# Two edits at the head of the routed blocks and one at the end of an attention, feed-forward and expert kernel

## The chip, the cores and the metric

The kernel runs on one core of a Trainium2 chip. The metric is the device time of one launch in microseconds (us). Engines are called by the names of the profile: PE is the matrix engine (PEld its weight loads), DVE is VectorE, ACT is ScalarE, POOL is GpSimd, and SP is SyncE, which here only issues transfers. A "q" behind the name of an engine (POOLq, DVEq, SPq) marks what its sequencer does alone: branches, register operations, waits, issues of transfers.

## The reference

Three stages follow one another on 2304 tokens (4 batches of 576) of 512 numbers, all in float32.

1. Attention of 8 heads of 64 with a causal window of 64 positions.
2. A dense feed-forward layer, 512 to 2048 to 512, with the activation h * tanh(softplus(h)).
3. A routed layer of 8 experts:

```python
do_compute = x @ w_skip > 0
xc = x[do_compute]
e_idx = argmax(xc @ w_gate)            # one expert of eight for each token
gate_w = softmax(xc @ w_gate)[e_idx]
for e in range(8):
    y[e_idx == e] = gate_w * (relu(xc @ w1[e]) @ w2[e])   # 512 -> 1024 -> 512
out = x;  out[do_compute] = xc + y
```

How many tokens an expert gets is known only on the chip, once the last token has been routed.

## The kernel before, in words

**Attention and dense layer** run in nine chunks of 256 tokens, each in eight ticks (`NC`, `NJ`); `tick(J)` of each engine says in which order it does its part. A chunk's result goes to `ytile`, SP stores it to `out` (`store_y`, line 407) and, with the gate in column 513, to the scratch tensor `y_rows` (`store_rows`, line 416). For each chunk the router finds expert and position of every token, and POOL scatters the token numbers into eight lists in DRAM (`scatter_tokens`, line 1505; `all_placed`, line 1516, waits until they have landed).

**Routed blocks.** A block is 128 tokens of one expert. PE makes the product with `w1` (`expert_up`, line 674, 64 matmuls of 128x128, 4 per 128 of the 1024 hidden numbers) in two halves, transposes the rows of the next block (`rows_T`, line 667, 4 matmuls), and makes the product with `w2` (`expert_down`, line 688). There `w2` and the hidden numbers are split into a rounded part and a rest (hi and lo), so that 24 matmuls of 128x512 add up in the bank `OB`. Around PE, in each engine's own order:

- ACT (`expert_block`, line 994) rounds the four quarters of `w2` (`split_w2`, line 872), makes the two halves of the ReLU (`expert_relu`, 886) and copies the next block's transposed rows (`rows_T_out`, 866).
- DVE (line 1427) takes the four rests of `w2` (`rest_of_w2`, 1240), the two rests of the ReLU (`rest_of_relu`, 1248), and writes gate times product plus row to `ot` (`gate_rows`, 1258).
- SP (`load_block`, line 433) reads the expert's number from a table in SBUF and issues two transfers of 2 MB: `w1` once the up product two blocks back is done (`bh_ok`), `w2` once the down product two blocks back is done (`bz_ok`). Each has two buffers, by the parity of the block. `w2_lo` lies over `w2`: the rests are written in place.
- POOL (line 1613) waits until the previous block's result has landed in `out` (`o_out`), loads the token numbers of the block three ahead (`load_tokens`, 1605), gathers the rows of the block two ahead into `xs` (`gather`, 1533), and scatters this block's result (`scatter_rows`, 1592). It does these one after the other.

**Blocks 0, 1 and 2 are early.** Their experts are picked before the last chunk is routed (`pick_first`, `pick_second`, `pick_third`, lines 1190 to 1238), on the experts' counts so far. So their weights and rows come while the last chunk is in work. All blocks from 3 on need the table `eid_i` and `row0_i`, which DVE computes after the last chunk (lines 1387 to 1422); the 20th step of the semaphore `tstep` says that it is there. Which expert each block has follows from the table; the experts that were not picked come in ascending order behind the early three.

**Order around the change.** SP (lines 470 to 488): `w1` of block 2; the last chunk's stores; `w2` of block 2 (after block 0's down product, since it goes to block 0's buffer); the wait for `tstep`; a wait for block 3's gathered rows (line 481); blocks 3 to 7; and then a loop over blocks 8 to 27, in which each block stands under a guard `If(i * RING + n < nblk)`, four guards to an iteration (`RING`), side by side. `nblk`, the number of blocks, is 12 on this input, so the loops of SP, PE, ACT, DVE and POOL run four iterations with sixteen false guards behind block 11. POOL (lines 1584 to 1624): the gather of block 2, the last chunk's token scatters, block 0's result, the wait that these tokens are placed, the wait for `tstep`, block 3's token numbers (1620), then `expert_block(1)`, with the numbers of block 4, the gather of block 3 and the result of block 1; behind the loop POOL waits for the landing of the last result (1624) and leaves. DVE, in the last tick (1300 to 1304), picks the third expert, takes two rests of block 1's `w2` and a rest of block 0's ReLU; then it copies the second half of the last chunk out of the bank `Y1` (1374, 1375), which PE's transposes and SP's stores wait for.

## Time and profile before

| what | us |
|---|---|
| median of three runs (722.07 to 725.32) | 723.67 |
| the profiled execution, its own time | 722.84 |
| span of the profiled execution, first to last instruction | 721.3 |
| of it, PE busy with matmuls (95%) | 684.9 |
| first matmul of the up product of block 2 | 565.32 |
| the same of block 4 | 604.14 |
| last matmul of block 11 begins | 709.22 |

All starts are counted from the start of the span. The time of an execution is 1.54 us more than its span. The mean granted clock of PE is 0.981 of full speed; a granted clock of 1.00 is 2.4 GHz and 0.50 is 1.2 GHz. A view called timeline lists instructions in order of their start, merged where they repeat; behind a row stands in brackets how long the engine had been idle and which instruction ended that. "Issue" there is time in which it waited for nothing that the profile shows.

### The profile page before, as it was taken

The numbers are of one execution on the slowest core, as the hardware profiler recorded it, in microseconds if no ns is written. First come the engines' busy times: TensorE is split into PE (matmuls) and PEld (weight loads), VectorE is DVE, ScalarE is ACT, GpSimd is POOL, SyncE is SP. The second block draws the span as 40 slices with busy tenths as digits, with TensorE's granted clock in tenths as the row PEclk, the third lists the DMA queues.
The fourth block names the chain that finished last, engine by engine and source line by source line (L and its number), as shares of the span: only waits on it lengthen the run. The fifth ranks groups of instructions, "written<-read, shape, count | busy, mean of one in ns | idle before, by whom it ended". The sixth has DMA issues, their size and how long they took to land. (4 is left out here: it accounts for less than half of the span.)

```text
span 721.3 us, 13783 instructions
## 1 busy us (share of the span) xinstructions
PE 684.9 (95%) x4958; PEld 605.2 (84%) x4958; DVE 489.0 (68%) x935; ACT 357.2 (50%) x784; POOL 253.7 (35%) x231
## 2 busy tenths in 40 slices
PE   5899999999999999999999999999999969999993
PEld 4776898888889888889889898988888868899992
DVE  5898767866866876785886785787788524364450
ACT  4546565555554654555555456544452323443430
POOL 4312434343443352443353353454652310221220
PEclk8999999999999999999999999999999998999998
DMA  9733221171164141232133124013477599999930
GB/s 273 236 117 118 74 67 37 39 126 44 37 119 98 48 96 37 75 70 63 42 91 75 37 46 124 1 31 94 174 289 217 163 393 333 343 330 354 349 126 2
DMA packets 62834, 97.16 MB, mean 135 GB/s; under 512 B 23014, under 2 KB 27110, under 8 KB 62768
## 3 DMA queue, kind: packets, MB, share of 16 engines
q1 hardware_dynamic: 59152, 91.01, 41.8%
q0 software_dynamic: 3168, 4.51, 1.9%
q10 hardware_dynamic: 448, 0.79, 0.4%
q8 instruction: 39, 0.64, 0.4%
q14 instruction: 27, 0.22, 0.2%
HBM read 84.97 MB, written 13.73 MB: 137 GB/s over the span
## 5 line engine op out<-in xcount | busy, mean ns | idle before, releaser
L1496 POOL TENSOR_TENSOR q_sb<-n_sb,r_sb 128x512 f32<-128x512 f32 x72 | 94.3, 1309 | 286.9 <-DVE a_sb L1101 162.9
L591 PE MATMUL Y<-wout_hi,g_hi 128*128 128x512 f32 x272 | 111.6, 410 | 3.2 <-ACT g_hi L845 3.0
L572 PE MATMUL H<-x_hi,win_hi 128*128 128x256 f32 x384 | 112.0, 292 | 2.0 <-DVE x_lo L1035 1.9
L572 PE MATMUL H<-x_hi,win_lo 128*128 128x256 f32 x384 | 108.4, 282 | 0.0
L572 PE MATMUL H<-x_lo,win_hi 128*128 128x256 f32 x384 | 108.4, 282 | 0.0
L591 PE MATMUL Y<-wout_lo,g_hi 128*128 128x512 f32 x272 | 107.3, 394 | 0.0
L684 PEld LDWEIGHTS H<-xT,w 128*128 128x128 f32 x768 | 89.2, 195 | 5.1 <-DMA w<-moe_w 4.2
L684 PE MATMUL H<-xT,w 128*128 128x128 f32 x768 | 89.7, 278 | 3.8 <-DMA w<-moe_w 3.8
L1502 POOL TENSOR_TENSOR g_lo<-g_sb,g_hi 128x512 fp32r<-128x512 f32 x68 | 88.3, 1298 | 2.5 <-ACT g_hi L845 1.9
L1081 DVE TENSOR_SCALAR u_sb<-e_sb 128x512 f32<-128x512 f32 x72 | 34.3, 476 | 71.9 <-ACT e_sb L830 71.2
L845 ACT CAST g_hi<-g_sb 128x512 fp32r<-128x512 f32 x68 | 42.2, 620 | 75.8 <-DVE g_sb L1114 75.4
L591 PE MATMUL Y<-wout_hi,g_lo 128*128 128x512 f32 x272 | 74.6, 396 | 1.4 <-POOL g_lo L1502 1.4
L572 PEld LDWEIGHTS H<-x_hi,win_hi 128*128 128x128 f32 x384 | 73.0, 190 | 3.2 <-DVE x_lo L1035 2.1
L572 PEld LDWEIGHTS H<-x_lo,win_hi 128*128 128x128 f32 x384 | 73.2, 191 | 0.8 <-issue 0.2
L572 PEld LDWEIGHTS H<-x_hi,win_lo 128*128 128x128 f32 x384 | 73.0, 190 | 0.0
L883 ACT CAST w_hi<-w 128x1024 fp32r<-128x1024 f32 x48 | 47.0, 1044 | 46.5 <-DMA w<-moe_w 46.5
L1245 DVE TENSOR_TENSOR w_lo<-w,w_hi 128x1024 fp32r<-128x1024 f32 x48 | 56.2, 1228 | 15.3 <-ACT w_hi L883 15.2
L591 PEld LDWEIGHTS Y<-wout_hi,g_hi 128*128 128x128 f32 x272 | 51.1, 188 | 16.1 <-ACT g_hi L845 6.3
L837 ACT ACTIVATE r_sb<-n_sb,two 128x512 f32<-128x512 f32 x72 | 51.9, 721 | 24.8 <-DVE n_sb L1086 24.6
L591 PEld LDWEIGHTS Y<-wout_hi,g_lo 128*128 128x128 f32 x272 | 50.8, 187 | 14.4 <-POOL g_lo L1502 2.1
L591 PEld LDWEIGHTS Y<-wout_lo,g_hi 128*128 128x128 f32 x272 | 51.2, 188 | 9.2
L572 PE MATMUL PTB<-x_hi,win_hi 128*128 128x256 f32 x192 | 55.3, 288 | 0.0
(196 smaller groups left out, 1402.8 us busy)
## 6 DMA issues: line engine op xcount, KB each, us to landing
w<-moe_w SPq DMA_DIRECT2D x24, 2048.0 KB, 11.1
kT<-k_T SPq DMA_DIRECT2D x32, 256.0 KB, 3.3
vw<-v_w SPq DMA_DIRECT2D x32, 256.0 KB, 3.1
y_rows<-ytile SPq DMA_DIRECT2D x36, 128.2 KB
out_rows<-ytile SPq DMA_DIRECT2D x36, 128.0 KB
win<-moe_w_in SPq DMA_DIRECT2D x8, 512.0 KB, 8.7
qbd<-q_T SPq DMA_DIRECT2D x64, 64.0 KB, 2.7
wout<-moe_w_out SPq DMA_DIRECT2D x8, 512.0 KB, 7.5
```

The source lines that it names most:

```text
L572: last = nc.tensor.matmul(HM3[J % 3][:, f, :], wt[:, j, d, f * P:(f + 1) * P], xt[:, c % 2, d, :], start=(n == 0), stop=(n == 3 * DB - 1))
L591: last = nc.tensor.matmul(Y[t][:, :], gt[:, J % 2, lo:lo + P], wt[:, 2 * j + f, :], start=(j == 0 and f == 0 and wt is wout_hi and gt is g ...
L684: last = nc.tensor.matmul(H[half][:, f * P:(f + 1) * P], w1[:, par, o:o + P], xT[:, par, d, :], start=(d == 0), stop=(d == DB - 1))
L837: nc.scalar.activation(r_sb[:, J % 2, :], n_sb[:, J % 2, :], ACT.Ln, bias=two[:, 0:1]).then_inc(t_ok, 1)
L845: nc.scalar.copy(g_hi[:, J % 2, :], g_sb[:, :]).then_inc(ghi_ok, 1)
L883: nc.scalar.copy(w2_hi[par][:, k * 1024:(k + 1) * 1024], w2[:, par, k * 1024:(k + 1) * 1024])\
L1081: nc.vector.tensor_scalar(u_sb[:, :], e_sb[:, :], EXP10, 2.0, ALU.min, ALU.add).then_inc(u_ok, 1)
L1245: nc.vector.tensor_tensor(w2_lo[:, par, at], w2[:, par, at], w2_hi[par][:, at].bitcast(FP32), ALU.subtract)\
L1496: nc.gpsimd.tensor_tensor(q_sb[:, :], n_sb[:, J % 2, :], r_sb[:, J % 2, :], ALU.mult).then_inc(q_ok, 1)
L1502: nc.gpsimd.tensor_tensor(g_lo[:, J % 2, :], g_sb[:, :], g_hi[:, J % 2, :].bitcast(FP32), ALU.subtract)\
```

## The change

**Block 3 early.** DVE gets four more steps after the third pick, `lowest_left`: the lowest of the experts not picked is the expert of block 3. SP loads its `w1` and `w2` before the wait for `tstep`, and POOL loads the first 128 numbers of its list and gathers its rows before that wait too. SP's wait for `xs_in[3]` is gone. PE turns (transposes) block 3's rows in the middle of block 2's down product, not ahead of it.

**A third buffer for block 2's `w2`.** `w2t` (with `w2t_lo` over it) lies over the dense weights and is loaded as soon as the dense layer's last product is done, ahead of the last chunk's stores; so block 3's `w2` is the first transfer that the odd buffer gets after block 1, and block 2 uses neither.

**DVE's order.** The copy out of `Y1` comes ahead of the second rest of block 1's `w2` and of block 0's second ReLU rest.

**Guards and end.** On every engine the four guards of an iteration are nested: if the first is false the other three aren't evaluated. The wait for the last result moves from POOL to DVE, which then multiplies one column of `ot`.

```diff
     def blocks(eng, nblk, block_of):
             with eng.Fori(NE // RING, LOOPS) as i:
-                for n in range(RING):
-                    with eng.If(i * RING + n < nblk):
+                with ExitStack() as guards:
+                    for n in range(RING):
+                        guards.enter_context(eng.If(i * RING + n < nblk))
                         block_of(i * RING + n, i, n)
...
+        def w2_there(eng, b, bh, slot_):
+            if third(b):                      # third(b): b == 2
+                eng.wait_ge(w2t_in, 16)
+            elif slot_ % 2 == 0 and not (isinstance(b, int) and b == 0):
+                eng.wait_ge(w2_in[0], loaded(bh, slot_) - 16)
+            else:
+                eng.wait_ge(w2_in[slot_ % 2], loaded(bh, slot_))
...
 SP
             sp.wait_ge(fixed, FSTEPS)
-            third = early_expert(2)
-            load_w1(third, 0)
+            e3 = early_expert(2)
+            load_w1(e3, 0)
+            sp.wait_ge(g2_ok, NJ * NC)
+            load_w2t(e3)
             sp.wait_ge(y1_ok, 1)
             store_y(NC - 1)
             store_rows(NC - 1)
-            sp.wait_ge(bz_ok, 1)
-            load_w2(third, 0)
+            sp.wait_ge(lowest, LSTEPS)
+            e4 = early_expert(EARLY)
+            sp.wait_ge(bh_ok, 4)
+            load_w1(e4, 1)
+            sp.wait_ge(bz_ok, 2)
+            load_w2(e4, 1)
             sp.wait_ge(tstep, TSTEPS)
             nblk = sp.value_load(cbi_i[0:1, NV - 1:NV], min_val=NE, max_val=NBLK)
-            sp.wait_ge(xs_in[EARLY], 16)
-            for b in range(EARLY, NE):
+            for b in range(EARLY + 1, NE):
                 load_block(b, b // RING, b % RING)
...
 PE
             def expert_block(b, bh, slot_):
                 for half in range(2):
                     expert_up(b, bh, slot_, half)
+                mid = EFB // 2 if third(b) else 0
+                if mid:
+                    expert_down(b, slot_, 0, mid)
                 rows_T(b + 1, bh + (slot_ + 1) // RING, (slot_ + 1) % RING)
-                expert_down(b, slot_, 0, EFB)
+                expert_down(b, slot_, mid, EFB)
...
 DVE
+            def lowest_left():
+                step, count = steps(lowest, 0)
+                atmax = df[:, 1, :]
+                step(nc.vector.tensor_tensor(atmax, early[:, :], rev[:, 0, :], ALU.mult))
+                step(nc.vector.reduce_max(turn[:, 0:1], atmax, AX.X))
+                step(nc.vector.tensor_scalar(early_e[:, EARLY:EARLY + 1], turn[:, 0:1], -1.0, float(NE), ALU.mult, ALU.add))
+                step(nc.vector.tensor_scalar(early_row[:, EARLY:EARLY + 1], turn[:, 0:1], -float(NTOK), float(NE * NTOK),
+                                             ALU.mult, ALU.add))
...
                 if c == NC - 1 and j == 7:
                     pick_third()
                     rest_of_w2(1, 1, 0)
-                    rest_of_w2(1, 1, 1)
-                    rest_of_relu(0, 1)
...
             dve.wait_ge(g2_ok, NJ * NC)
             nc.vector.tensor_copy(ytile[:, (NC - 1) % 2, 1, 0:D], Y[1][:, :]).then_inc(y1_ok, 1)
+            rest_of_w2(1, 1, 1)
+            rest_of_relu(0, 1)
             dve.wait_ge(ytr_ok, NC * 2)
             nc.vector.tensor_copy(q_sb[:, :], PTB[:, :]).then_inc(yT1_ok, 1)
+            lowest_left()
             rest_of_w2(1, 1, 2)
...
             blocks(dve, nblk, expert_block)
+            dve.wait_ge(o_out, nblk * 16)
+            nc.vector.scalar_tensor_tensor(out=ot[:, 0, 0:1], in0=ot[:, 0, 0:1], scalar=two[:, 0:1], in1=ot[:, 0, 0:1],
+                                           op0=ALU.mult, op1=ALU.add)
...
 POOL
             scatter_rows(0, 0)
             all_placed(NC - 1)
+            pool.wait_ge(lowest, LSTEPS)
+            load_early(EARLY)
+            pool.wait_ge(y_out[0], 128 * 6)
+            gather(0, EARLY)
             pool.wait_ge(tstep, TSTEPS)
             nblk = pool.value_load(cbi_i[0:1, NV - 1:NV], min_val=NE, max_val=NBLK)
...
                 pool.wait_ge(o_out, b * 16)
                 load_tokens(b + 3, after(bh, slot_, 3)[1])
-                gather(*after(bh, slot_, 2))
+                if not (isinstance(b, int) and b == 1):
+                    gather(*after(bh, slot_, 2))
                 scatter_rows(b, slot_)
 
-            load_tokens(3, 3)
-            pool.wait_ge(y_out[0], 128 * 6)
             expert_block(1, 0, 1)
             blocks(pool, nblk, expert_block)
-            pool.wait_ge(o_out, nblk * 16)
```

`load_w2t` is `load_w2` into `w2t`, with the semaphore `w2t_in`; `split_w2`, `rest_of_w2` and `expert_down` read and write `w2t` and `w2t_lo` for block 2 in place of `w2` and `w2_lo`.

## Rows read from the trace of the kernel before

**Rows 1.** Timeline of PE, 545 to 618 us: start, duration, line, operation [idle before <-releaser].

```profile
545.59 0.66 PE L620 MATMUL PTB<-ident,ytile 128*128 128x128 f32 x4 [0.80 <-DVE ytile L1375]
...
565.32 7.30 PE L684 MATMUL H<-xT,w 128*128 128x128 f32 x64
572.84 0.66 PE L671 MATMUL SB_<-ident,xs 128*128 128x128 f32 x4 [0.22 <-DMA xs<-y_rows,blk_tok]
...
583.32 9.04 PE L684 MATMUL H<-xT,w 128*128 128x128 f32 x64 [3.76 <-DMA w<-moe_w]
...
595.80 0.76 PE L702 MATMUL OB<-w_hi,hT_hi 128*128 128x512 f32 x1 [3.00 <-DVE hT_lo L1255]
...
604.14 7.31 PE L684 MATMUL H<-xT,w 128*128 128x128 f32 x64
611.29 0.60 PE L671 MATMUL SB_<-ident,xs 128*128 128x128 f32 x4
...
617.28 7.31 PE L684 MATMUL H<-xT,w 128*128 128x128 f32 x64
```

**Rows 2.** Windows: length, busy time and instructions of each engine, PEclk, DMA share, GB/s.

```profile
565.00:570.00 5.00, 5.00 (x45) 4.91 (x44) 2.35 (x3) 2.68 (x3) 2.11 (x3) 1.00 0.07 22
```

**Rows 3.** The same view, block 3.

```profile
583.30:604.10 20.80, 17.78 (x92) 15.86 (x93) 5.83 (x6) 8.81 (x11) 1.60 (x2) 0.75 1.03 398
```

**Rows 4.** Waits of SP's queue: engine, line <- waited for: total, times, longest.

```profile
SPq L434 <- DMA xs<-y_rows,blk_tok: 10.1, 1, 10.1
```

**Rows 5.** Timeline of SP: issue of block 3's first matrix.

```profile
573.52 0.38 SPq L427 DMA_DIRECT2D w<-moe_w  x1
```

**Rows 6.** Timeline of DVE around the last chunk's copy.

```profile
540.73 0.17 DVE L1231 TENSOR_TENSOR taken<-taken,pos 128x8 f32<-128x8 f32 x1
540.93 0.17 DVE L1232 TENSOR_TENSOR early<-early,ohe 128x8 f32<-128x8 f32 x1
...
541.97 2.36 DVE L1245 TENSOR_TENSOR w_lo<-w,w_hi 128x1024 fp32r<-128x1024 f32 x2
...
544.85 0.68 DVE L1375 COPY ytile<-Y 128x512 f32<-128x512 f32 x1
```

**Rows 7.** Timeline of POOL: list and gather of block 3, and steady pairs.

```profile
565.91 0.58 POOL L1607 DMA_DIRECT2D blk_tok<-tokens_of_experts  x1 [7.68 <-DMA out_rows<-ot,blk_tok]
...
569.03 1.52 POOL L1537 DMA_INDIRECT xs<-y_rows,blk_tok  x1 [1.35 <-DMA blk_tok<-tokens_of_experts]
...
606.03 1.15 POOL L1595 DMA_INDIRECT out_rows<-ot,blk_tok  x1 [15.14 <-DVE ot L1264]
...
614.88 1.05 POOL L1537 DMA_INDIRECT xs<-y_rows,blk_tok  x1 [0.31 <-issue]
```

**Rows 8.** Source views: landing times of the token lists (L1607).

```profile
DMA to landing us min/median/max: 2.3/5.3/6.4
```

**Rows 9.** The same for the gathers (L1537).

```profile
DMA to landing us min/median/max: 2.1/5.9/7.2
```

**Rows 10.** The same for the result scatters (L1595).

```profile
DMA to landing us min/median/max: 2.3/6.9/8.0
```

**Rows 11.** Source view of L1603, POOL's load of the block count.

```profile
L1603 POOLq TENSOR_LOAD <-cbi_i x1: 300/300/300, 564.2 to 564.2; - x1
```

**Rows 12.** Timeline from 709.7 us, all engines: all that is left.

```profile
709.83 0.75 DVE L1264 SCALAR_TENSOR_TENSOR ot<-OB,xs 128x512 f32<-128x512 f32 x1 [4.90 <-PE OB L702]
711.44 1.01 POOL L1595 DMA_INDIRECT out_rows<-ot,blk_tok  x1 [7.59 <-DVE ot L1264]
```

**Rows 13.** POOL's guards, 711.4 to 712.3 (L320), and loop control, 709 to 722 (L318).

```profile
L320 POOLq COMPARE_BRANCH  x4: 45/45/50, 711.6 to 712.2; - x4
...
L318 POOLq FUSED_REGOPS  x4: 35/35/47, 711.5 to 714.8; - x4
```

**Rows 14.** Source view of L55, leaving the program: min/median/max ns, first and last start.

```profile
L55 POOLq COMPARE_BRANCH  x1: 38/38/38, 715.9 to 715.9; - x1
L55 POOLq DRAIN  x1: 4971/4971/4971, 716.1 to 716.1; - x1
```

More of the change, by code:

```diff
@@ L75, in build @@
         dv = sb("dv", [P, NV])
-        early_e = sb("early_e", [P, EARLY], I32)
-        early_row = sb("early_row", [P, EARLY], I32)
+        early_e = sb("early_e", [P, EARLY + 1], I32)
+        early_row = sb("early_row", [P, EARLY + 1], I32)
         turn = sb("turn", [P, EARLY])
@@ L185, in build @@
             cbi_i = sb("cbi_i", [P, NV], I32, exp_)
+            with ExitStack() as raw:
+                w2t = sb("w2t", [P, EFB * D], FP32, raw)
+            w2t_lo = sb("w2t_lo", [P, EFB * D], F32R, exp_)
         with ExitStack() as exp_:
@@ L251, in build @@
         fixed = sem("fixed")
+        lowest = sem("lowest")
         xz_ok = sem("xz_ok")
@@ L260, in build @@
         w2_in = [sem("w2_in0"), sem("w2_in1")]
+        w2t_in = sem("w2t_in")
         w2hi_ok = sem("w2hi_ok")
@@ L279, in build @@
         FSTEPS = 13
+        LSTEPS = 4
         block = ctx.enter_context(nc.Block())
@@ L318, in blocks, with third, w2_raw, w2_rest @@
             with eng.Fori(NE // RING, LOOPS) as i:
-                for n in range(RING):
-                    with eng.If(i * RING + n < nblk):
+                with ExitStack() as guards:
+                    for n in range(RING):
+                        guards.enter_context(eng.If(i * RING + n < nblk))
                         block_of(i * RING + n, i, n)
+        def third(b):
+            return isinstance(b, int) and b == 2
+        def w2_raw(b, slot_):
+            return w2t[:, :] if third(b) else w2[:, slot_ % 2, :]
+        def w2_rest(b, slot_):
+            return w2t_lo[:, :] if third(b) else w2_lo[:, slot_ % 2, :]
+        def w2_there(eng, b, bh, slot_):
[5 more added lines that the diff above has]
+                eng.wait_ge(w2_in[slot_ % 2], loaded(bh, slot_))
         def loaded(bh, slot_):
@@ L431, in load_w2, with load_w2t @@
                 sp.dma_start(w2[:, par, :].rearrange("p (f n) -> p f n", f=EFB), e2).then_inc(w2_in[par], 16)
+            def load_w2t(e):
+                e2 = w2_dram[bass.ds(e, 1), :, :].rearrange("o (f p) n -> p (o f) n", p=P)
+                sp.dma_start(w2t[:, :].rearrange("p (f n) -> p f n", f=EFB), e2).then_inc(w2t_in, 16)
             def load_block(b, bh, slot_):
@@ L476, in _ @@
             store_rows(NC - 1)
-            sp.wait_ge(bz_ok, 1)
-            load_w2(third, 0)
+            sp.wait_ge(lowest, LSTEPS)
[4 more added lines that the diff above has]
+            load_w2(e4, 1)
             sp.wait_ge(tstep, TSTEPS)
             nblk = sp.value_load(cbi_i[0:1, NV - 1:NV], min_val=NE, max_val=NBLK)
-            sp.wait_ge(xs_in[EARLY], 16)
-            for b in range(EARLY, NE):
+            for b in range(EARLY + 1, NE):
                 load_block(b, b // RING, b % RING)
             with sp.Fori(NE // RING, LOOPS) as i:
-                for n in range(RING):
-                    with sp.If(i * RING + n < nblk):
+                with ExitStack() as guards:
+                    for n in range(RING):
+                        guards.enter_context(sp.If(i * RING + n < nblk))
                         load_block(i * RING + n, i, n)
@@ L699, in expert_down @@
                         pe.wait_ge(hTlo_ok[f // 4], b + 1)
-                    for hT, wt in ((hT_hi, w2_hi[par][:, f * D:(f + 1) * D]), (hT_hi, w2_lo[:, par, f * D:(f + 1) * D]),
+                    for hT, wt in ((hT_hi, w2_hi[par][:, f * D:(f + 1) * D]), (hT_hi, w2_rest(b, slot_)[:, f * D:(f + 1) * D]),
                                    (hT_lo, w2_hi[par][:, f * D:(f + 1) * D])):
@@ L875, in split_w2 @@
                 if k == 0:
-                    act.wait_ge(w2_in[par], loaded(bh, slot_))
+                    w2_there(act, b, bh, slot_)
                     if isinstance(b, int) and b == 0:
@@ L882, in split_w2 @@
                         act.wait_ge(bz_ok, b - 1)
-                nc.scalar.copy(w2_hi[par][:, k * 1024:(k + 1) * 1024], w2[:, par, k * 1024:(k + 1) * 1024])\
+                nc.scalar.copy(w2_hi[par][:, k * 1024:(k + 1) * 1024], w2_raw(b, slot_)[:, k * 1024:(k + 1) * 1024])\
                     .then_inc(w2hi_ok, 1)
@@ L1238, in pick_third @@
                 assert count[0] == FSTEPS, count
+            def lowest_left():
[6 more added lines that the diff above has]
+                                             ALU.mult, ALU.add))
+                assert count[0] == LSTEPS, count
             def rest_of_w2(b, slot_, k):
@@ L1244, in rest_of_w2 @@
                 at = slice(k * 1024, (k + 1) * 1024)
-                nc.vector.tensor_tensor(w2_lo[:, par, at], w2[:, par, at], w2_hi[par][:, at].bitcast(FP32), ALU.subtract)\
+                nc.vector.tensor_tensor(w2_rest(b, slot_)[:, at], w2_raw(b, slot_)[:, at], w2_hi[par][:, at].bitcast(FP32),
+                                        ALU.subtract)\
                     .then_inc(w2lo_ok, 1)
```

## The prediction

> **What bounds the kernel now.** PE is busy for 684.9 of 721.3 us, so the end moves only with PE's idle stretches, with its clock, and with what comes after its last matmul. I read the timeline of PE first, to find where it stands still behind the dense layer [rows 1]. Block 4 starts its up product at 604.14 and block 5 at 617.28: a block takes 13.14 us when nothing is late. Blocks 2 and 3 take 604.14 - 565.32 = 38.82 us where 26.28 would do, 12.54 us too much. In them PE waits 0.22 us for block 3's rows, 3.76 us for block 3's `w1` and 3.00 us for the rest of its ReLU, and its clock falls after it has stood: the mean granted clock over block 3 is 0.75, a mixture of 2.4 and 1.2 GHz [rows 3]. Ahead of that, a wait of 0.80 us for the copy out of `Y1` is PE's only other one here [rows 1].
>
> Who made `w1` late is read from SP's waits: 10.1 us on the gathered rows of block 3 [rows 4], after which it issues `w1` at 573.52 [rows 5] and PE can start at 583.32 [rows 1], 9.8 us later. Meanwhile the DMA engines stood almost idle, with a share of 0.07 between 565 and 570 us [rows 2]. So a wait, not bandwidth, held block 3's weights back. The rows themselves were late since POOL read the list at 565.91 and gathered at 569.03 [rows 7].
>
> The tail is the second place. DVE's last result starts at 709.83 and POOL's scatter at 711.44 [rows 12]; the span goes on to 721.3. The scatter lands 2.3 us after its start, the minimum of its kind [rows 10], at 713.7. But POOL reaches its wait only at 715.9, where it passes within 0.04 us, and then needs a DRAIN of 4.97 us [rows 14]. What fills 711.5 to 715.7 are the guards [rows 13]. The tail is thus guards plus DRAIN, and the landing is covered by the guards.
>
> **DVE's order.** The copy out of `Y1` loses two instructions ahead of it: it started at 544.85 and could start when the first of the two rests is done, at 541.97 + 1.18 = 543.15, so 1.7 us sooner [rows 6]. PE's wait was 0.80 us and ends whole: the copy would now be done a little before PE asks. The displaced rests are needed by `OB` products that come several microseconds later, so they cost nothing. Blocks 1 and 2 begin 0.80 us sooner, block 2 at 564.52. The four steps of `lowest_left` start 0.20 us apart [rows 6], 0.8 us in all; they stand where DVE waits for the logits, and PE gives the logits at its own pace, so I take nothing. Uncovered they would cost 0.8 us of the router, not of PE, since PE has block 1 to do meanwhile.
>
> **Block 3's weights.** SP's order is now `w1` and `w2t` of block 2 (4 MB), eight stores, then `w1` of block 3 once block 1's up product is done. That is 564.52 less the 5.9 us of a down product with its transposes (13.14 - 7.15, less rounding) [rows 1], so about 558.6. With the 9.8 us of the old one it is there by 568.4, 9 us ahead of need. `w2` follows at 564.5; were it to need 12 us behind `w1` it would land at 576.5, and PE's down product of block 3 begins at 585 or later. Rounding and rests fit between. `w2t` removes block 2's late split: it is issued near 542.5, some 15 us before ACT can use it. The whole excess of 12.54 us is thus freed, if nothing else comes late: 13.34 us with the 0.80. The stores behind `w2t` are later by the time of one 2 MB transfer; only block 3's gather waits for them, and it stands behind more than that.
>
> **What is late next: block 3's rows.** POOL still reads the list after the last tokens are placed. That read was at 565.91 [rows 7]. It moves up by 0.80 us with the router and by the load of the block count, now behind it: 0.30 us for the load [rows 11] and, as an estimate, 0.2 us for the register work with it. So 564.6. The old read landed in 2.3 us, with the DMA engines idle [rows 2, 8]. Now `w1` and then `w2` of block 3 are on the way, as in the steady blocks, so I take the median of 5.3 us [rows 8]: 569.9. POOL starts the gather 569.03 - 565.91 - 2.3 = 0.8 us behind a landing [rows 7]: 570.7. It lands at the median of 5.9 us [rows 9]: 576.6. PE asks for the rows 7.15 us into block 2 (611.29 - 604.14) plus half of the 24 matmuls, 2.8 us of the remaining 5.6 us: at 564.52 + 9.95 = 574.5. So it waits 2.1 us in mid-product. The bounds are no wait (2.3 and 2.1 us of landing, the minima) and 4.5 us (6.4 and 7.2 us) [rows 8, 9].
>
> The page "DMA: Bandwidth & Descriptors" of the Trainium skill, section "Anatomy of one DMA — SWDGE (gpsimd) path", prices a transfer issued by GpSimd at about 2.0 us plus its bytes over 436 GB/s, an estimate of 2.6 us for this gather of 0.26 MB. By it the rows would land in time and the sum would be 2.1 us less; the median of the rows in this loaded stretch disagrees.
>
> **The second lateness.** POOL works in order. Behind the gather at 570.7 it needs 1.05 us for it, 0.9 us for block 4's list with its gap, and 0.3 us: block 1's result leaves at 572.9 where 566.4 would be usual (1.9 us into the block, 606.03 against 604.14) [rows 1, 7]. It lands after 6.9 us, the median [rows 10], and the gather of block 4 follows 614.88 - 606.03 - 6.9 = 1.95 us later, at 581.8, landing at 587.7. Block 3 starts at 564.52 + 13.14 + 2.1 = 579.8 and asks at 586.9: 0.8 us. One block on, POOL is back in step by the same count, and the loss ends. Bounds: 0 and 3 us. PE's waits together are 2.9 us, and blocks 2 and 3 give back 13.34 - 2.9 = 10.4 us.
>
> **The tail.** Guards follow one another by 0.22 us (four in 711.6 to 712.2), and an iteration takes 1.10 us (four loop controls from 711.5 to 714.8) [rows 13]. Nested, three of four aren't evaluated: 0.66 us less in each of four iterations, 2.6 us. True guards cost what they did. POOL then leaves the loop at 713.3 in place of 715.9 and, with no wait, begins its DRAIN at 713.4. If that takes the same 4.97 us [rows 14], the end comes 2.65 us sooner. DVE's wait ends with the landing at 713.7 and its one-column multiply takes some 0.2 us: covered by the DRAIN, as is the landing. What the DRAIN waits for no row shows. It began 2.3 us after everything had landed and still took 4.97 us, so I take it as fixed from its start; the bounds are a gain of nothing (its end is tied to the last scatter) and of 7.3 us (it vanishes, and the landing ends the program).
>
> **Sum.** Against the profiled execution's own 722.84 us: -13.34, +2.9, -2.65 give 709.8. That execution is 0.8 us below the median of 723.67, so 710.6 by the median; I round it down to 710, since the next likeliest case lies below.
>
> **Rivals.**
> - *No wait for rows* (0.24). The list or the gather lands like the better ones, and PE goes through: 722.84 - 13.34 - 2.65 = 706.9, or 707.7 by the median. For it: the first of the two reads is issued with a single transfer in flight; against it: both medians.
> - *The tail gives nothing* (0.17), because the DRAIN ends a fixed time after the last scatter or because the guards compile to what they were: 710.6 + 2.65 = 713.3.
> - *A longer wait in mid-product, and the clock with it* (0.14). Idle for 3.76 us, PE went on at 1.2 GHz and took 9.04 instead of 7.31 us for the next product [rows 1]. With a wait of 4.5 us and such a fall, 1.7 to 4 us more: 714 to 717. Waits of up to 0.80 us left the clock at 1.00; where between it turns, the rows don't say.
> - *Leaving the guards costs a fetch* (0.04). A nested false guard jumps over four bodies at once. If each such jump had to fetch its target with a transfer on idle DMA engines, 2.3 us by the shortest landing [rows 8], four would put 9.2 us behind POOL's last scatter, and the time by the median would be 710.6 + 9.2 = 719.8. Against it: before, sixteen jumps over single bodies show no gap. The Trainium skill's page "Runtime: NRT & Kernel Launch", section "Instruction fetch mechanics", has the rule: a taken branch whose target isn't in the two pages at hand must wait for a fetch.
> - *Slower* (0.03). PE waits in mid-product at the lower clock and keeps it: the ask at 574.5 is missed by over 4.5 us, and blocks 2 to 4 run at 1.2 GHz, where a block takes up to 13.1 us more. It decides from 20 us of such losses on, one and a half blocks at the low clock: 727. Against it, block 3 was back at 2.4 GHz before its end even after two waits of over 3 us.
>
> **How the numbers follow.** My forecast has 0.38. A change of 0.5% (3.6 us) is about what a measurement of this kernel tells from none. The forecast, the first two rivals, and the long wait all end more than that below 723.67; the fetch lies at its edge, the last one beyond. That makes 0.93 faster, 0.04 within, 0.03 slower. The range of 706 to 715 leaves out the worst of the long wait, the last two rivals, and a DRAIN that vanishes.
>
> **What would show it.** Right: block 2 starts near 564.5 with no wait for `Y1`; PE waits for `xs` in mid-product by 0 to 4.5 us and for no `w`; block 4 starts at 591 to 596; SP has no wait at line 434 on `xs`; POOL's guards end near 2.6 us after they begin less than now, and a DRAIN of about 5 us starts without a wait. Wrong: a wait of PE for `w` or `hT_lo` in block 3, a clock of 0.50 anywhere behind 565, or a DRAIN that begins sooner and ends where it did.

## The result, and the profile after

The changed kernel takes 716.49 us, the median of 20 runs (713.52 to 723.02), against 722.72 of the kernel before (20 runs, 719.67 to 727.17): a ratio of 0.9918, 95% interval 0.9897 to 0.9939. It is 6.2 us faster. I had forecast 710.0 with a range of 706 to 715: the sign was right, the gain less than half of what I said (6.2 us where I had 13.7), and the value lies outside the range. The profiled execution of the changed kernel took 717.35 us, with a span of 715.7.

The span by itself misleads here, since the two profiled executions differ before the first changed instruction. The page of the changed kernel, part 2:

```profile
PE   6898999989999999999999999999999799999995
...
PEclk9899999998999999999999999999999999999998
DMA  9734231161236134115114214102637989999940
```

The tenth digit of the clock, an 8 (161 to 179 us), is not in the page of before: there the granted clock of this stretch was 1.00, here 0.87, at 1.2 GHz for some microseconds after PE had waited for POOL in the dense layer. In the view of waits, 100 to 200 us of the changed kernel, that one is (engine, tile, line <- waited for: total, times, longest)

```profile
PE Y L627 <- POOL g_lo L1557: 2.6, 1, 2.6
```

In the kernel before the same wait was 1.37 us and the clock stayed up. So I count from a mark that lies behind the dense layer, the first transposes of the last chunk's result (`y_T`), called **the mark** below. It stood at 544.19 us in the trace before. The timeline of PE after, the same columns as in [rows 1]:

```profile
549.27 0.60 PE L656 MATMUL MB<-ident,ytile 128*128 128x128 f32 x4
...
556.17 7.39 PE L720 MATMUL H<-xT,w 128*128 128x128 f32 x64
567.49 0.66 PE L707 MATMUL SB_<-ident,xs 128*128 128x128 f32 x4 [3.93 <-DMA xs<-y_rows,blk_tok]
...
575.13 7.31 PE L720 MATMUL H<-xT,w 128*128 128x128 f32 x64
...
588.27 7.31 PE L720 MATMUL H<-xT,w 128*128 128x128 f32 x64
...
601.46 7.31 PE L720 MATMUL H<-xT,w 128*128 128x128 f32 x64
```

Block 1 starts 6.90 us behind the mark; before it was 552.11 - 544.19 = 7.92. The wait for the copy out of `Y1` is gone. Block 4 starts at 601.46 - 549.27 = 52.2 us, against 604.14 - 544.19 = 60.0. In between PE waits for no `w` and for no ReLU rest. But it waits 3.93 us for the rows of **block 2**, which were in time before, and then goes on at 1.2 GHz for a while, as the windows show (length, busy times, PEclk, DMA share, GB/s):

```profile
556.00:568.00 12.00, 8.07 (x73) 7.78 (x72) 9.06 (x34) 1.19 (x2) 4.88 (x4) 1.00 1.08 321
568.00:572.00 4.00, 4.00 (x13) 3.14 (x12) 0.00 (x0) 3.54 (x5) 0.00 (x0) 0.57 0.94 270
```

The wait's cause stands in the queues. First the timeline of SP, 547 to 564 us of the changed kernel, then that of POOL, 557 to 578 us. SP puts 4 MB ahead of the stores, and the first four stores take 6.58 us to issue, where the trace before has 2.43 us. POOL's gather of block 2 (L1592, 557.79) starts while the last of the four `y_rows` stores is being issued:

```profile
547.82 0.38 SPq L453 DMA_DIRECT2D w<-moe_w  x1
548.30 0.45 SPq L461 DMA_DIRECT2D w2t<-moe_w  x1
548.91 6.58 SPq L439 DMA_DIRECT2D out_rows<-ytile  x4
555.67 2.38 SPq L448 DMA_DIRECT2D y_rows<-ytile  x4
563.73 0.39 SPq L453 DMA_DIRECT2D w<-moe_w  x1
```

```profile
557.79 1.08 POOL L1592 DMA_INDIRECT xs<-y_rows,blk_tok  x1 [5.27 <-DVE slot L1212]
559.17 1.02 POOL L1566 DMA_INDIRECT tokens_of_experts<-tok_i,slot  x1 [0.30 <-issue]
560.50 1.80 POOL L1566 DMA_INDIRECT tokens_of_experts<-tok_i,slot  x1 [0.31 <-issue]
562.61 0.97 POOL L1650 DMA_INDIRECT out_rows<-ot,blk_tok  x1 [0.30 <-issue]
572.27 0.58 POOL L1580 DMA_DIRECT2D blk_tok<-tokens_of_experts  x1 [8.69 <-issue]
577.03 1.52 POOL L1592 DMA_INDIRECT xs<-y_rows,blk_tok  x1 [4.18 <-issue]
```

By the source view of its line the gather of block 2 landed after 9.7 us, its maximum. In the trace before the same gather, 7.8 us behind the mark where it is 8.5 here, landed after 4.1 us.

The tail did what was said. The timeline from 706.5 us, then the source view of L55 (leaving the program) and that of L327 (the guards), 708 to 711 us, each with min/median/max ns and the first and last start:

```profile
706.53 0.40 PE L738 MATMUL OB<-w_hi,hT_lo 128*128 128x512 f32 x1
707.14 0.75 DVE L1315 SCALAR_TENSOR_TENSOR ot<-OB,xs 128x512 f32<-128x512 f32 x1 [4.90 <-PE OB L738]
708.75 1.02 POOL L1650 DMA_INDIRECT out_rows<-ot,blk_tok  x1 [7.54 <-DVE ot L1315]
711.04 0.22 DVE L1488 SCALAR_TENSOR_TENSOR ot<-ot,two 128x1 f32<-128x1 f32 x1 [3.15 <-DMA out_rows<-ot,blk_tok]
```

```profile
L55 POOLq DRAIN  x1: 4971/4971/4971, 710.5 to 710.5; - x1
```

```profile
L327 POOLq COMPARE_BRANCH  x4: 45/45/50, 708.9 to 710.2; - x4
```

Four guards are evaluated where there were sixteen, 0.45 us apart (708.9 to 710.2, three gaps), against 1.10 us for an iteration of four [rows 13]. The DRAIN begins at 710.5, ahead of the landing, and takes 4.971 us again. From the start of the last matmul to the end of the span it is 715.7 - 706.5 = 9.2 us, before 721.3 - 709.2 = 12.0.

### The profile page after: what moved, and what is told of

Same layout as the page of the kernel before. It is cut to its first block, busy times and chain, and to the rows that moved or that the text cites. A ratio compares the mean times of both kernels' runs of the same rounds, so it can differ in the third digit from the quotient of the medians.

```text
span 715.7 us, 13644 instructions
## 1 busy us (share of the span) xinstructions
PE 684.7 (96%) x4958; PEld 605.9 (85%) x4958; DVE 488.9 (68%) x940; ACT 357.6 (50%) x784; POOL 255.2 (36%) x231
## 4 chain that ended last, share of the span: by engine, by line
PE 79%; DVE 8%; DMA 5%; issue 3%; ACT 2%; POOL 1%; SPq 1%; POOLq 0%; DVEq 0%; ACTq 0%
PE Y L627 22%; PE H L608 16%; PE H L720 10%; PE OB L738 10%; PE PTB L608 8%; PE SB_ L573 4%; PE OB L592 2%; PE MB L668 2%; PE SB_ L581 2%; DMA tokens_of_experts<-tok_i,slot 1%; DMA xs<-y_rows,blk_tok 1%; DVE a_sb L1140 1%; DVE u_sb L1120 1%; PE Y L641 1%; PE MB L656 1%
## 5 line engine op out<-in xcount | busy, mean ns | idle before, releaser
L720 PEld LDWEIGHTS H<-xT,w 128*128 128x128 f32 x768 | 87.6, 192 | 1.0
L720 PE MATMUL H<-xT,w 128*128 128x128 f32 x768 | 88.0, 275 | 0.0
L608 PE MATMUL PTB<-x_hi,win_hi 128*128 128x256 f32 x192 | 55.3, 288 | 0.0
L608 PE MATMUL PTB<-x_hi,win_lo 128*128 128x256 f32 x192 | 54.0, 281 | 0.0
L1295 DVE TENSOR_TENSOR w_lo<-w,w_hi 128x1024 fp32r<-128x1024 f32 x44 | 51.7, 1229 | 3.3 <-ACT w_hi L922 3.2
## 6 DMA issues: line engine op xcount, KB each, us to landing
w<-moe_w SPq DMA_DIRECT2D x23, 2048.0 KB, 10.3
```

What stands on the lines that cost most here:

```text
L608: last = nc.tensor.matmul(HM3[J % 3][:, f, :], wt[:, j, d, f * P:(f + 1) * P], xt[:, c % 2, d, :], start=(n == 0), stop=(n == 3 * DB - 1))
L720: last = nc.tensor.matmul(H[half][:, f * P:(f + 1) * P], w1[:, par, o:o + P], xT[:, par, d, :], start=(d == 0), stop=(d == DB - 1))
L1295: nc.vector.tensor_tensor(w2_rest(b, slot_)[:, at], w2_raw(b, slot_)[:, at], w2_hi[par][:, at].bitcast(FP32), ALU.subtract)\
```

## The experiments

Three theories stood against each other. **Traffic:** what the change loads earlier shares the DMA engines with the small dependent transfers (list and gather of block 2; token scatter, list, gather of block 3) and slows those. **Chance or POOL:** the wait was one execution's, or POOL simply asks late. **Dense layer:** what is missing from my forecast is no part of the change. All traces, in the order in which they were taken ("wait" is PE's longest between mark and block 4; tail is from the last matmul's start to the end of the span):

| kernel | mark, us | block 4 behind it | longest wait, for | tail |
|---|---|---|---|---|
| before | 544.2 | 60.0 | 3.76, `w1` of block 3 | 12.0 |
| changed | 549.3 | 52.2 | 3.93, rows of block 2 | 9.2 |
| changed, again | 544.7 | 54.3 | 5.89, rows of block 3 | 9.2 |
| w2t after block 2's rows | 544.0 | 54.1 | 4.97, ReLU rest of block 2 | 9.2 |
| w2t after the stores | 545.9 | 52.5 | 4.24, rows of block 2 | 9.2 |
| guards side by side | 544.8 | 53.7 | 5.05, rows of block 3 | 11.8 |
| little of block 3's weights | 553.5 | 53.6 | 5.19, rows of block 2 | 9.2 |
| turned ahead | 548.2 | 55.3 | 5.83, rows of block 2 | 9.2 |
| turned later | 549.0 | 53.7 | 5.26, rows of block 2 | 9.2 |
| w2 of block 3 behind its list | 550.8 | 52.3 | 2.86, rows of block 3 | 9.2 |
| z1 | 551.0 | 53.1 | 2.47, ReLU rest of block 3 | 9.2 |
| z2 | 545.8 | 50.5 | 1.55, ReLU rest of block 3 | 9.2 |
| before, guards nested | 546.0 | 58.1 | 3.62, `w1` of block 3 | 9.9 |
| changed, last wait on POOL | 549.8 | 54.6 | 5.63, rows of block 2 | 9.9 |
| z3 | 543.9 | 48.0 | 0.83, ReLU rest of block 3 | 9.2 |
| changed, third trace | 545.0 | 52.6 | 4.44, rows of block 2 | 9.2 |
| before, again | 546.3 | 56.0 | 3.48, `w1` of block 3 | 12.0 |

**The changed kernel again** (no edit).

> The changed kernel once more, as it is, to see which of its waits return. Traffic theory (the transfer of w2t and the eight stores behind it share the DMA engines with the list and the gather of block 2, which so take 9.7 us instead of 4.1): PE again waits 3 to 5 us for block 2's rows, and no wait for them is seen for block 3. Rival (chance: that wait was one execution's): under 1 us. Third theory (the dense layer was unlucky in the profiled execution: a wait of 2.6 us for g_lo at 158 us and 6.8 us at 1.2 GHz behind it, some 4.4 us of the 13 I had forecast): the first transposes of the last chunk's result start nearer 544.2, as before, than 549.3.

714.82 us, ratio 0.9910 (0.9882 to 0.9938). The dense part is quick here. Now PE waits 5.89 us for block 3's rows and for none of block 2's. Its timeline of PE, then that of POOL:

```profile
558.81 0.60 PE L707 MATMUL SB_<-ident,xs 128*128 128x128 f32 x4
...
564.79 7.30 PE L720 MATMUL H<-xT,w 128*128 128x128 f32 x64
...
580.77 1.12 PE L707 MATMUL SB_<-ident,xs 128*128 128x128 f32 x4 [5.89 <-DMA xs<-y_rows,blk_tok]
...
585.77 7.31 PE L720 MATMUL H<-xT,w 128*128 128x128 f32 x64
```

```profile
552.43 1.08 POOL L1592 DMA_INDIRECT xs<-y_rows,blk_tok  x1 [4.88 <-issue]
...
555.21 0.99 POOL L1566 DMA_INDIRECT tokens_of_experts<-tok_i,slot  x1 [0.30 <-issue]
...
568.18 0.58 POOL L1580 DMA_DIRECT2D blk_tok<-tokens_of_experts  x1 [10.47 <-issue]
573.94 1.05 POOL L1592 DMA_INDIRECT xs<-y_rows,blk_tok  x1 [5.18 <-issue]
```

Neither expectation was met as written: there is one wait of 4 to 6 us, but for either block. The gather of block 2 started 7.7 us behind the mark here, landed after 6.1 us and was in time. Block 3's chain is 13.0 us from the second token scatter to the list, 5.8 to the gather and 6.8 to PE. The two waits hide one another. PE, where it has lost nothing before, asks for block 3's rows 30.2 us behind the mark; in this trace they land at 36.0. In the first trace they landed at 34.9 (the gather at 577.03 and 7.1 us), but there PE asked only at 35.8, having lost 5.6 us over block 2's.

**w2t later.**

```diff
-            sp.wait_ge(g2_ok, NJ * NC)
-            load_w2t(e3)
             sp.wait_ge(y1_ok, 1)
             store_y(NC - 1)
             store_rows(NC - 1)
+            sp.wait_ge(xs_in[2], 16)       # left out in "after the stores"
+            load_w2t(e3)
```

> The changed kernel with w2t loaded only after block 2's rows have landed. Traffic theory: PE's wait for block 2's rows falls to under 1 us and the clock doesn't fall there; w2t lands some 9 us behind those rows, block 2's split then ends just in time, a wait of 0 to 2 us for it or for block 3's rows. Block 4 starts 3 to 5.5 us sooner, counted from the first transposes of the last chunk. Rival (the rows are late since POOL asks late, whatever else is on the way): the wait stays at 3 to 5 us.

> The changed kernel with w2t behind the last chunk's eight stores, as w2 of block 2 was before the change, at about 10 us behind the first transposes. Traffic theory: the gather of block 2 is in flight at that time with the stores alone, as before: its wait is under 1 us. If it is the stores and not w2t that delay the rows, the wait stays at 2 us or more here too. Block 4 starts 3 to 5.5 us sooner by the traffic theory, the same by the rival that POOL asks late.

Behind block 2's rows: 713.85 us, ratio 0.9881 (0.9835 to 0.9927). The wait for block 2's rows is gone, as the traffic theory says, but w2t now lands too late and PE waits 4.97 us for `hT_lo`: block 4 at 54.1, not the 3 to 5.5 us sooner that were expected. Behind the stores alone: 714.85 us, ratio 0.9913 (0.9886 to 0.9940), and the wait stays, 4.24 us, although the stores had room before w2t. There w2t is issued 0.2 us behind the gather. So it isn't the stores' place in the queue that decides, but the 2 MB on their way when the gather reads. The other traces bear it out. In the four with w2t behind the rows (this one, z1, z2, z3) the gather started 8.4 to 10.1 us behind the mark, SP, which waited for its landing, issued w2t 4.2 to 4.8 us later, and PE had no wait for it. In the ten with w2t at its place or right behind the stores, it started at 7.3 to 9.4 and PE waited for it in eight. There its landing grew with its start: some 6 us in the two that started by 7.8, 8.0 at 7.9, and 9.7 to 11.1 in the seven from 8.5 on. In the three traces of the kernel before, the same 2 MB were issued 0.9 to 2.1 us behind the gather, and PE waited for it in none.

The token scatters show the same. From the second of them to block 3's list it is 3.7 to 5.2 us in those four kernels and 8.8 to 13.0 in the ten.

**Little of block 3's weights on the way.** `w1` of block 3 only for one of four groups of rows, `w2` when block 3's rows have landed; the kernel leaves out three quarters of that `w1`, so block 3's products use block 1's weights there.

```diff
-            load_w1(e4, 1)
+            load_w1_part(e4, 1)            # [:, 0:1, :] of the four groups
             sp.wait_ge(bz_ok, 2)
+            sp.wait_ge(xs_in[EARLY], 16)
             load_w2(e4, 1)
```

> The changed kernel with almost nothing of block 3's weights on the way while its rows are fetched: a quarter of its w1 is loaded (three quarters of that product's weights are left as block 1's) and its w2 only when its rows have landed. In the changed kernel run again, the last tokens landed 11.7 us after their scatter, the list 4.9 and the rows 6.8 us after theirs, and PE stood 5.9 us in mid-product. If the early weights are what slows this chain: the tokens land within 9 us, the list within 3 and the rows within 4.5 us of their issues, and PE's wait for the rows is under 1 us (a late w2 then makes it stand in block 3 instead). If the chain is slow by itself or by w2t and the stores: tokens still over 10 us, and the wait stays over 3 us.

One execution, 723.0 us, with the mark at 553.5. List and rows met the expectation (landings of 2.3 and 3.5 us), the tokens did so at its edge. POOL's timeline of this kernel (L1585 is its list, L1597 its gather):

```profile
565.26 1.32 POOL L1571 DMA_INDIRECT tokens_of_experts<-tok_i,slot  x1 [0.31 <-issue]
...
575.58 0.58 POOL L1585 DMA_DIRECT2D blk_tok<-tokens_of_experts  x1 [7.73 <-issue]
578.67 1.05 POOL L1597 DMA_INDIRECT xs<-y_rows,blk_tok  x1 [2.50 <-issue]
```

From the list to the gather 3.1 us, as before, 569.03 - 565.91 = 3.1 [rows 7]; the two traces of the changed kernel above have 577.03 - 572.27 = 4.8 and 5.8. From the second token scatter to the list 10.3 us, against 11.8 and 13.0; but with all of `w1` it is 10.6 and 10.9 in two of the traces below, so `w1` isn't shown to slow the tokens. PE's wait for block 3's rows is nothing, but block 2's rows, with w2t and stores beside them, cost 5.19 us. List and gather of block 3 are thus slowed by its weights, block 2's gather and the tokens by w2t and the stores.

**Where block 3's rows are turned.** All of the down product behind the transposes, or more of it ahead.

```diff
-                mid = EFB // 2 if third(b) else 0
+                mid = 0                        # ahead
+                mid = 6 if third(b) else 0     # later
```

> The changed kernel with the turning of block 3's rows ahead of block 2's down product again, all else as it is. If the rows come when they come (35 to 36 us behind the first transposes of the last chunk): PE stands 2.8 us longer there, and block 4 starts 2.8 us later, plus up to 1 us of clock. If block 2's rows are the ones that are late in this execution, no wait for block 3's rows and no difference.

> The changed kernel with block 3's rows turned behind six eighths of block 2's down product, not four. If PE's wait there is set by the landing of the rows: it is 1.4 us shorter, and block 4 starts 1.4 us sooner, or more if the clock then stays up; the copy of the turned rows still hides behind the last 6 matmuls (1.4 us). Against that, ACT's split of w2 begins later by as much, with no wait to be seen. If something else ended the wait, no difference.

Ahead: 719.85 us, ratio 0.9933 (0.9901 to 0.9966); later: 718.82 us, 0.9941 (0.9903 to 0.9979). In both traces block 2's rows were the late ones, 5.83 and 5.26 us, and nothing was left to wait for at block 3's. So they tell little of the turning: block 4 at 55.3 is above, 53.7 within what the unedited kernel shows. I count both as inconclusive.

**w2 of block 3 behind its list.**

```diff
             sp.wait_ge(bz_ok, 2)
+            sp.wait_ge(bt_in[EARLY], 16)
             load_w2(e4, 1)
```

> The changed kernel with w2 of block 3 issued only when the list of block 3 has landed. Theory that weights on the way slow the chain: list 2 to 3 us sooner, so PE's wait for the rows shrinks by 2 to 3 us; w2 lands near 580 to 582 and may cost up to 2 us in block 3's product. If the token scatters are the slow part (they are over by then, and w1 is what runs beside them): nothing is gained, and up to 2 us lost.

719.14 us, ratio 0.9932 (0.9887 to 0.9977). Waits of 1.67 (block 2's rows) and 2.86 us (block 3's), none with a fall of the clock, but 0.64 more for block 4's rows: block 4 at 52.3, within the changed kernel's spread. The list took 4.2 us, where it takes 4.9 in the trace of the changed kernel that has `w2` ahead of it: 0.7 us, not the 2 to 3 expected. `w2` then meets the gather, which took 7.4 us against 6.8 to 7.2.

**The tail, piece by piece.** The first edit puts the guards of the changed kernel back side by side, the second nests those of the kernel before and changes nothing else, the third moves the last wait back to POOL.

```diff
 changed, guards side by side (the kernel before, guards nested: the reverse)
-                with ExitStack() as guards:
-                    for n in range(RING):
-                        guards.enter_context(eng.If(i * RING + n < nblk))
+                for n in range(RING):
+                    with eng.If(i * RING + n < nblk):
...
 changed, last wait on POOL
-            dve.wait_ge(o_out, nblk * 16)
-            nc.vector.scalar_tensor_tensor(out=ot[:, 0, 0:1], in0=ot[:, 0, 0:1], scalar=two[:, 0:1], in1=ot[:, 0, 0:1],
-                                           op0=ALU.mult, op1=ALU.add)
...
+            pool.wait_ge(o_out, nblk * 16)
```

> The changed kernel with the four guards side by side again, the last wait still on DVE. If the guards are 2.6 us of the tail and the DRAIN of 4.97 us starts at their end whatever it is: from the last matmul to the end of the span 11.4 us, against 8.8 in the changed kernel. If the DRAIN is tied to the last scatter: 8.8 us still. DVE's own guards end near 5.6 us behind its last result, so it isn't last.

> The kernel before with nested guards alone, the last wait still on POOL. POOL leaves its guards 1.8 us after it enters them instead of 4.3, meets a landing that comes 2.3 us after the scatter, and begins its DRAIN then: from the start of the last matmul to the end of the span 12.0 - 2.2 = 9.8 us. If the DRAIN is tied to the scatter, 12.0. Blocks 2 and 3 as before: block 4 near 60 us behind the first transposes of the last chunk, if the profiled execution was typical.

> The changed kernel with the last wait back on POOL, guards nested. POOL's DRAIN begins at the landing, some 0.4 to 0.6 us later than the end of its guards: the tail is 9.6 to 9.9 us against 9.2. If the DRAIN is the longer the sooner it begins: 9.2 still.

11.8, 9.9 and 9.9 us. The differences are as expected; the first value is 0.4 above its 11.4, as the changed kernel's 9.2 is above the 8.8 that it was set against. Nesting takes 12.0 to 9.9 on the kernel before, and 11.8 to 9.2 on the changed one; moving the wait takes 9.9 to 9.2. Timed, the side-by-side guards gave 716.81 us, ratio 0.9939 (0.9911 to 0.9965). The DRAIN is 4971 ns in all of these traces, whatever its start. The source view of L55, first of the changed kernel with side-by-side guards, then of the kernel before with nested ones:

```profile
L55 POOLq DRAIN  x1: 4971/4971/4971, 710.1 to 710.1; - x1
```

```profile
L55 POOLq DRAIN  x1: 4971/4971/4971, 713.8 to 713.8; - x1
```

**Three versions that order the work by its need.** z1 is "w2t after block 2's rows", and ACT and DVE take block 2's ReLU halves ahead of the quarters of w2t that come late. z2 also holds block 3's `w1` until the tokens are placed. z3 does for block 3 what was done for block 2.

```diff
 ACT, and DVE in the same order with rest_of_relu and rest_of_w2
             def expert_block(b, bh, slot_):
+                if third(b):                                   # z1, z2, z3
+                    for half in range(2):
+                        expert_relu(b, half)
+                        split_w2(b, bh, slot_, 2 * half)
+                        split_w2(b, bh, slot_, 2 * half + 1)
+                elif isinstance(b, int) and b == 3:            # z3
+                    for half in range(2):
+                        split_w2(b, bh, slot_, 2 * half)
+                        split_w2(b, bh, slot_, 2 * half + 1)
+                        expert_relu(b, half)
...
 SP
             sp.wait_ge(bh_ok, 4)
+            sp.wait_ge(placed, NC + 2)                         # z2, z3
             load_w1(e4, 1)
...
 PE
-                mid = EFB // 2 if third(b) else 0
+                mid = EFB // 2 if isinstance(b, int) and b in (2, 3) else 0    # z3
```

> Two edits on the changed kernel. w2t is loaded only when block 2's rows have landed, as in the run that moved only this; there PE had 4.97 us to wait for block 2's rounding instead. And for block 2 ACT and DVE take each half of the ReLU ahead of two quarters of w2t, not behind all four, so that PE's down product can start with the first quarter. Traffic theory: no wait for block 2's rows, 1 to 2 us in block 2's product, 0 to 2 us for block 3's rows; block 4 starts 48 to 50 us behind the first transposes of the last chunk, against 52.2 to 54.3 so far. Rival (whatever is freed ahead, the rows of block 3 land 36 us behind those transposes and set the end): 52 or more.

> As the one before, and w1 of block 3 is issued only when the last tokens have been placed. Traffic theory: tokens and list land 1 to 3 us sooner, w1 still in time (needed some 33 us behind the transposes); block 4 starts at 47 to 49 us. Rival: the token scatters are slow by themselves, w1 is only later: no better than the one before, or worse by up to 2 us.

> As z2, and for block 3 too the product is started with what is there: ACT and DVE take the first half of its ReLU behind two quarters of its w2, and block 4's rows are turned in mid-product. z2 still lost 1.0 us waiting for block 4's rows and 1.55 us waiting for the rest of block 3's ReLU. If the loss is a matter of order: both waits are under 0.3 us, block 4 starts 47.3 to 49 us behind the first transposes of the last chunk (z2 50.5), and the time is 2 to 6 us below the changed kernel's on this chip. If it is a bound of the round trips: the wait moves to block 4's or 5's rows, and block 4 or 5 starts no sooner than in z2.

z1: 714.12 us, ratio 0.9859 (0.9811 to 0.9907). Its block 3 starts 34.7 us behind the mark (changed kernel 39.0 and 41.1), but block 3 then lacks its own ReLU rest: block 4 at 53.1, by the rival's number and not by its mechanism. z2: 717.22 us, 0.9890 (0.9843 to 0.9938); its trace is better (50.5) than z1's, its time isn't. It misses the expected 47 to 49, and holding `w1` did nothing for the tokens: 4.8 us from the scatter to the list, z1 4.1. Its waits were 1.00 us for block 4's rows and 1.55 for block 3's ReLU rest. z3 takes the first away and leaves 0.83 us of the second, where under 0.3 was expected. Its timeline of PE (L721 the up products of blocks 2 to 4, L708 the transposes of block 3's rows, L739 block 3's down product), then that of POOL (L1589 the second token scatter, L1603 block 3's list, L1615 its gather):

```profile
564.04 7.30 PE L721 MATMUL H<-xT,w 128*128 128x128 f32 x64
...
574.39 0.66 PE L708 MATMUL SB_<-ident,xs 128*128 128x128 f32 x4 [0.26 <-DMA xs<-y_rows,blk_tok]
...
577.66 7.31 PE L721 MATMUL H<-xT,w 128*128 128x128 f32 x64
...
585.80 0.47 PE L739 MATMUL OB<-w_hi,hT_hi 128*128 128x512 f32 x1 [0.83 <-DVE hT_lo L1318]
...
591.90 7.31 PE L721 MATMUL H<-xT,w 128*128 128x128 f32 x64
```

```profile
555.01 1.97 POOL L1589 DMA_INDIRECT tokens_of_experts<-tok_i,slot  x1 [0.31 <-issue]
...
560.20 0.58 POOL L1603 DMA_DIRECT2D blk_tok<-tokens_of_experts  x1 [1.94 <-issue]
568.01 1.05 POOL L1615 DMA_INDIRECT xs<-y_rows,blk_tok  x1 [7.23 <-issue]
```

708.12 us (706.57 to 710.18), ratio 0.9821 (0.9796 to 0.9845); block 4 at 591.90 - 543.94 = 48.0 us, as expected. The list is asked for 5.2 us behind the scatter, w2t having been issued only 2.1 us behind it, and then takes 7.8 us to the gather, with w2t and `w1` beside it. On the same chip

> The changed kernel as it is, on the same chip as z3. Block 4 starts 52 to 54.5 us behind the transposes, with a wait of 4 to 6 us for the rows of block 2 or of block 3; the tail is 9.2 us. By the theory of a race: if the gather of block 2 starts before 8 us behind the transposes (ahead of the y_rows stores) it lands within 6 us and block 3's rows are what PE waits for; if later, it takes 10 us and PE waits for block 2's.

the changed kernel took 713.88 us, ratio 0.9911 (0.9882 to 0.9941), with its wait for block 2's rows (gather at 8.7 us, landing 10.0 us later). z3 is thus clear of both kernels: its slowest run is faster than the changed kernel's fastest (712.75).

> The kernel before as it is, for one more look at its blocks 2 and 3. If its profiled execution was typical: block 4 at 59.5 to 60.5 us behind the transposes, a wait of 3.5 us and more for w1 of block 3 and one of 3 us for its ReLU, clock at 1.2 GHz for some 10 us. If that execution was dear: 56 to 58.5.

The kernel before, once more: 721.0 us, the mark at 546.3, and block 4 at 56.0. Its waits in blocks 2 and 3 are those of [rows 1], a little shorter, in its timeline of PE:

```profile
584.26 9.94 PE L684 MATMUL H<-xT,w 128*128 128x128 f32 x64 [3.48 <-DMA w<-moe_w]
...
596.67 0.47 PE L702 MATMUL OB<-w_hi,hT_hi 128*128 128x512 f32 x1 [2.03 <-DVE hT_lo L1255]
...
602.29 7.30 PE L684 MATMUL H<-xT,w 128*128 128x128 f32 x64
```

## Why the prediction was right and where it was wrong

**DVE's order: right.** PE's 0.80 us ended whole. The gain in the traces is 1.0 us (7.9 to 6.9 behind the mark).

**Block 3's weights: right, and SP's wait was the cause.** No trace of the changed kernel has PE waiting for `w1` or for block 3's ReLU rest.

**The tail: right.** 12.0 to 9.2 us, 2.65 forecast. The DRAIN is fixed from its start. The rule of the Trainium skill's page "Runtime: NRT & Kernel Launch", section "Instruction fetch mechanics", that a branch past the pages at hand waits for a fetch, changes nothing here: the nested false guards followed one another by 0.45 us, as the count from [rows 13] has it, with no gap that a fetch could fill. Whether their targets lie past those pages no run here shows.

**The step that failed: "only block 3's gather waits for them", and with it the two landings taken at the median.** I asked who waits for the stores, and not what else shares the engines with w2t. Block 2's gather does. It was in time before, I gave its lateness no term, and in three traces of the unedited changed kernel it cost 3.93, 0 and 4.44 us. Where it didn't, block 3's rows did, 5.89 us instead of my 2.1: its list was asked for 13.0 us behind the token scatter, where I had moved the old distance of 10.2 along (565.91 less the scatter at 555.7), although I changed what runs beside it. Behind the mark I had the list at 20.4 us (564.6 less 544.19); the changed kernel has it at 23.0 to 23.5 in all three traces, and that is most of what the rows came later. List and gather of block 3 kept within the steady blocks' bounds of 6.4 and 7.2 us (3.9 to 4.9, and 6.8 to 7.2, the upper end). Block 2's gather, up to 11.1 us, did not. The Trainium skill's page "DMA: Bandwidth & Descriptors", section "Anatomy of one DMA — SWDGE (gpsimd) path", gave an estimate of 2.6 us for a gather and is farther off still: of blocks 2 and 3 none landed under 3.5 us in any trace.

**The second lateness: not there.** I had 0.8 us for block 4's rows. PE waits for them in no trace of the changed kernel.

**The clock, too.** The rival "a longer wait in mid-product, and the clock with it" (0.14, 714 to 717 us) has the measured time, and its clock is in the traces: with each wait of 3.9 us and more the granted clock fell to 1.2 GHz, and PE worked on at it for 3.3 to 6.0 us. Half of that stretch is lost. But its wait in mid-product, for block 3's rows, is in one of the three traces of the changed kernel; in the other two PE stood ahead of block 1's down product, for block 2's, which no rival names. That the number fits is in part luck.

**The sizes.** Measured by the mark, the changed kernel starts block 4 at 52.2, 54.3 and 52.6 us, and at 53.7 and 54.6 with other guards and the other last wait, which don't act there: a mean of 53.5. I had 60.0 - 10.4 = 49.6: 3.9 us of the miss. The rest is the base. Three traces of the kernel before (one with nested guards, which don't act there) have 60.0, 58.1 and 56.0, a mean of 58.0: my one execution held 2.0 us more excess than usual. That its total was ordinary all the same came from a cheap dense part: its mark at 544.2 is 1.8 us ahead of the median of the 17 traces, 546.0. Together 5.9 of the 6.7 us between 709.8 and 716.5; for the last 0.8 no run shows a cause, and the means, of three traces with a spread of 4.0 us and of five with 2.4, are no better known than that. That I rounded the sum of 710.6 down to 710 had no ground.

The dense part's spread of marks (543.9 to 553.5) goes with the wait at 158 us, for POOL and behind it for a token transfer: it is 2.6 us and more in the seven traces with the mark at 548 or later, and at most 1.8 in the ten others. That it is the cause isn't shown; I made no run on it.

## What to carry to other kernels

- A transfer made earlier is paid by the small dependent ones beside it. List for the stretch into which it moves every transfer in flight, above all chains of scatter, list and gather, and price each link with that company, not with its old distance or with the steady loop's.
- A load is best issued by when it is needed, not as soon as it can be: z3 gained 5.8 us on the changed kernel (713.88 to 708.12) by holding two loads back and starting products with what was there. What each of its edits gave isn't told apart; holding w2t alone only moved PE's wait (block 4 at 54.1).
- One profiled execution is a sample in both of its parts: compare from a mark behind the unchanged work, and let an engine with a long fixed exit leave first.

## What the runs showed of the hardware that I had not expected

- POOL's DRAIN at the end of the program took 4971 ns in all 17 traces, before or behind the landing of the last scatter; the same instruction of DVE took 17 ns in the kernel before, and 216 to 243 where DVE ends with its multiply.
- A gather of 128 rows of 2 KB landed after 3.8 us on almost idle DMA engines, after some 6 to 7 us in the steady blocks, and after up to 11.1 us with a 2 MB load, or 4 MB and eight stores, issued around it. Between two traces of the changed kernel a start 0.8 us later (8.5 in place of 7.7 us behind the mark) went with a landing 3.6 us slower, 9.7 against 6.1.
- With two 2 MB loads ahead in SP's queue, the issue of four 128 KB stores took 6.3 to 6.9 us instead of 2.4.
